# Two bursts of value products a batch instead of five, with readings and copies reordered

## What is computed

```python
scores = scale * np.matmul(q, k.transpose(0, 1, 3, 2)) + bias
attn = np.exp(scores - scores.max(-1, keepdims=True))
attn = attn / (attn.sum(-1, keepdims=True) + 1e-09)
attn_out = np.matmul(attn, v)
...
for e in range(E):
    out += P[:, e:e + 1] * (np.maximum(x @ w1[e], 0.0) @ w2[e])
```

## Time and profile before

| | |
|---|---|
| median of 3 runs | 1844.34 us (1844.29 to 1845.65) |
| the profiled execution | 1844.29 us |
| its span, first to last instruction | 1842.5 us |
| PE busy | 1826.9 us (99%), 10223 matmul records |
| DVE, ACT, POOL busy | 1054.5, 824.6, 1028.1 us |
| chain that ended last | PE 95%, DVE 1% |
| granted TensorE clock | 9 tenths or more in all 40 slices |

### The profile page before, as it was taken

One profiled execution on the slowest core, in us unless ns is written; L12 is line 12 of the kernel. 1 busy time (PEld: TensorE's weight loads), 2 busy tenths in 40 slices (PEclk: granted clock), 3 DMA queues, 4 the chain that ended last, 5 costly groups with the idle time before them and its releaser, 6 DMA issues.

```text
span 1842.5 us, 27892 instructions
## 1 busy us (share of the span) xinstructions
PE 1826.9 (99%) x10223; PEld 1590.0 (86%) x10223; DVE 1054.5 (57%) x1784; ACT 824.6 (45%) x1416; POOL 1028.1 (56%) x720
## 2 busy tenths in 40 slices
PE   8999999999999999999999999999999999999999
PEld 4677777798999999999999999999999999999998
DVE  8877777778554555456545554555465545544553
ACT  8877777533433333344333333333333333333331
POOL 0223326577666666666776666666666666666661
PEclk9999999999999999999999999999999999999999
DMA  7764562021111111112121122121121111111210
GB/s 229 243 150 97 129 148 68 23 92 53 65 67 69 69 69 69 69 69 103 69 69 69 69 69 69 69 69 69 70 103 69 69 69 69 69 69 69 69 46 35
DMA packets 44127, 152.47 MB, mean 83 GB/s; under 512 B 9584, under 2 KB 18032, under 8 KB 29680
## 3 DMA queue, kind: packets, MB, share of 16 engines
q1 hardware_dynamic: 44016, 150.99, 25.5%
HBM read 135.63 MB, written 15.34 MB: 82 GB/s over the span
## 4 chain that ended last, share of the span: by engine, by line
PE 95%; DVE 1%; ACT 0%; POOL 0%; issue 0%; POOLq 0%; DVEq 0%
PE banks L660 14%; PE banks L661 14%; PE banks L659 14%; PE banks L627 13%; PE banks L631 13%; PE banks L629 13%; PE banks L557 4%; PE banks L518 3%; PE banks L500 3%; PE banks L501 2%; PE banks L571 1%; PE banks L528 0%; PE banks L678 0%; ACT probs L786 0%; DVE x_lo_rest_r L1081 0%
## 5 line engine op out<-in xcount | busy, mean ns | idle before, releaser
L1279 POOL TENSOR_TENSOR w_lo<-stage,w_hi 128x1024 fp32r<-128x1024 f32 (+1 forms) x288 | 647.4, 2264 | 525.7 <-ACT w_hi L832 524.7
L1161 DVE TENSOR_TENSOR u<-p_copy,banks 128x384 f32<-128x384 f32 x192 | 106.3, 554 | 632.0 <-PE banks L631 632.0
L661 PE MATMUL banks<-w_hi,h_lo 128*128 128x512 f32 x1152 | 450.1, 391 | 0.0
L660 PE MATMUL banks<-w_lo,h_hi 128*128 128x512 f32 x1152 | 449.9, 391 | 0.0
L659 PE MATMUL banks<-w_hi,h_hi 128*128 128x512 f32 x1152 | 449.0, 390 | 0.0
L1167 DVE SCALAR_TENSOR_TENSOR h_lo<-corner,h_hi 128x384 fp32r<-128x384 f32 x384 | 412.7, 1102 | 0.0
L879 ACT ACTIVATE h_hi<-corner 128x384 fp32r<-128x384 f32 x384 | 196.5, 526 | 270.9 <-DVE corner L1161 267.9
L627 PE MATMUL banks<-x_hi,w_hi 128*128 128x384 f32 x896 | 300.6, 335 | 0.0
L631 PE MATMUL banks<-x_hi,w_lo 128*128 128x384 f32 x896 | 300.2, 335 | 0.0
L832 ACT ACTIVATE w_hi<-stage 128x1024 fp32r<-128x1024 f32 (+1 forms) x288 | 271.6, 974 | 8.8 <-POOL stage L1273 8.8
L868 ACT ACTIVATE p_copy<-banks 128x384 f32<-128x384 f32 x96 | 47.4, 493 | 491.0 <-PE banks L631 491.0
(11 more groups left out here) (130 smaller groups left out, 2472.2 us busy)
## 6 DMA issues: line engine op xcount, KB each, us to landing
stage<-in_expert_w SPq DMA_DIRECT2D x96, 1024.0 KB, 4.8
raw<-in_qk SPq DMA_DIRECT2D x32, 576.0 KB, 7.2
bias_scratch<-bias_out SPq DMA_DIRECT2D x36, 288.0 KB, 2.6
bias<-bias_scratch SPq DMA_DIRECT2D x16, 288.0 KB, 2.9
v_main<-in_v SPq DMA_DIRECT2D x16, 256.0 KB, 2.7
bias<-bias_scratch SPq DMA_DIRECT2D x16, 256.0 KB, 3.8
out<-total SPq DMA_DIRECT2D x4, 768.0 KB, 4.0
out<-total SPq DMA_DIRECT2D x6, 256.0 KB, 2.0
```

Of the source, the lines that this page charges most:

```text
L660: pe.matmul(dst, h_hi[:, g % 2, f, tokens], lo[:, f], start=False, stop=False)
L661: mm = pe.matmul(dst, h_lo[:, g % 2, f, tokens], hi[:, f], start=False, stop=fp == FPAIRS - 1 and f == 1)
L1161: dve.tensor_tensor(out, other, bank, op).then_inc(combined, 1)
L1279: pool.tensor_tensor(lo, of, hi.bitcast(F32), ALU.subtract).then_inc(w_split, 1)
```

## The change

The five parts of the value products become two: half 0 whole in step 4 after the transposes, half 1 whole in step 1 of the next batch, before them. VectorE reads half 0 first thing in step 0 (before: after row sums) and half 1 in step 1 between reductions and copies (before: step 3); it copies the rest before the second head's block in steps 2 and 3; the row sums and reciprocal come last in step 0. ScalarE copies between the two exponentials in step 0, and rounds both heads of the next pair in step 1, one before its copy and one after. No arithmetic is added or left out. `HEADS_AT` gives the steps after a batch's first at which its halves are read.

```diff
--- before.py
+++ after.py
@@ -58,9 +58,10 @@
 PIECES = len(PIECE_AT) - 1
 
 
-PV_PARTS = ((4, 0, range(0, 3), False), (5, 0, range(3, 5), True),
-            (6, 1, range(0, 2), False), (7, 1, range(2, 3), False), (8, 1, range(3, 5), True))
-PV_DONE = (2, 5)
+PV_PARTS = ((4, 0, range(0, 5), False), (6, 1, range(0, 5), True))
+PV_DONE = (1, 2)
+HEADS_AT = (5, 6)
+REST_FIRST = (2, 3)
 TAIL = 6
 TOK = N // P
 ITERS = 8
@@ -776,17 +777,21 @@
                     hidden_units(m + AHEAD, (m + AHEAD) % ROUND)
                 keep_bias(m, m % ROUND)
             def step(hp, s, last=False):
-                if exists(hp, s):
+                def exponentials(h):
+                    if not exists(hp, s):
+                        return
                     slot = batch(hp, s)[1]
                     rows = queries(s % QC)
-                    for h in range(2):
-                        act.wait_ge(biased, 2 * (hp * STEPS + s) + h + 1)
-                        row = probs[0:rows, s % 2, S * h:S * h + S]
-                        total_at = 2 * (s % QC) + h
-                        act.activation(row, row, ACT.Exp, bias=neg_max[0:rows, 2 * (s % 2) + h:2 * (s % 2) + h + 1],
-                                       scale=-1.0,
-                                       accum_out=row_sum[0:rows, slot, total_at:total_at + 1]).then_inc(exped, 1)
-                if exists(hp, s - 1):
+                    act.wait_ge(biased, 2 * (hp * STEPS + s) + h + 1)
+                    row = probs[0:rows, s % 2, S * h:S * h + S]
+                    total_at = 2 * (s % QC) + h
+                    act.activation(row, row, ACT.Exp, bias=neg_max[0:rows, 2 * (s % 2) + h:2 * (s % 2) + h + 1],
+                                   scale=-1.0,
+                                   accum_out=row_sum[0:rows, slot, total_at:total_at + 1]).then_inc(exped, 1)
+
+                def keep_turned():
+                    if not exists(hp, s - 1):
+                        return
                     at, rows = hp * STEPS + s - 1, queries((s - 1) % QC)
                     act.wait_ge(turned[0], at + 1)
                     q_at = (s - 1) % QC * P
@@ -796,6 +801,20 @@
                     act.activation(probs_t[:, 0:KC, q_at:q_at + rows],
                                    banks[:, 4, :].rearrange("p (c q) -> p c q", c=KC)[:, :, 0:rows],
                                    ACT.Copy).then_inc(kept_t[0], 1)
+
+                def round_next(h):
+                    if s % QC == 1 and exists(hp, s) and exists(hp, s - QC) and not (last and s // QC == B - 1):
+                        n, slot = batch(hp, s + QC)
+                        round_pair(n, slot, h)
+
+                exponentials(0)
+                if s % QC == 0:
+                    keep_turned()
+                exponentials(1)
+                round_next(0)
+                if s % QC != 0:
+                    keep_turned()
+                round_next(1)
                 first = not exists(hp, s - QC)
                 if s % QC == 0 and not first:
                     n, slot = batch(hp, s - QC)
@@ -805,9 +824,6 @@
                     act.activation(inv_wide[:].rearrange("p (r d) -> p r d", d=D),
                                    row_inv[:, slot, :].unsqueeze(2).broadcast_to([P, 2 * QC, D]),
                                    ACT.Copy).then_inc(inv_widened, 1)
-                if s % QC in (1, 2) and exists(hp, s) and not first and not (last and s // QC == B - 1):
-                    n, slot = batch(hp, s + QC)
-                    round_pair(n, slot, s % QC - 1)
             for s in range(STEPS):
                 step(0, s)
             with act.Fori(1, PAIRS - 1) as hp:
@@ -1027,6 +1043,12 @@
                 n, slot = batch(hp, s)
                 qc = s % QC
                 rows = queries(qc)
+
+                def heads_due(half):
+                    if (s - HEADS_AT[half]) % QC == 0 and exists(hp, s - HEADS_AT[half]):
+                        keep_heads(hp, s - HEADS_AT[half], half)
+
+                heads_due(0)
                 for h in range(2):
                     if exists(hp, s):
                         if s < QC and h == 0:
@@ -1044,6 +1066,21 @@
                         for piece in range(PIECES):
                             if (s - 8 - piece) % QC == 0 and exists(hp, s - 8 - piece):
                                 scale_heads(hp, s - 8 - piece, piece)
+                heads_due(1)
+                if exists(hp, s - 1):
+                    rows, q_at = queries((s - 1) % QC), (s - 1) % QC * P
+                    free = columns_free(hp, s - 1)
+                    if free is not None:
+                        dve.wait_ge(pv_done, free)
+                    for part in ((2, 1) if qc in REST_FIRST else (1, 2)):
+                        dve.wait_ge(turned[part], at)
+                        if part == 1:
+                            dve.tensor_copy(probs_t[:, KC:2 * KC, q_at:q_at + rows],
+                                            banks[:, 5, :].rearrange("p (c q) -> p c q", c=KC)[:, :, 0:rows]
+                                            ).then_inc(kept_t[1], 1)
+                        else:
+                            dve.tensor_copy(probs_t[:, 2 * KC, q_at:q_at + rows],
+                                            rest_bank[:, 0:rows]).then_inc(kept_t[2], 1)
                 if qc == 0 and exists(hp, s - QC):
                     n, slot = batch(hp, s - QC)
                     dve.wait_ge(exped, 2 * at)
@@ -1053,24 +1090,6 @@
                                       ALU.add).then_inc(inv_step, 1)
                     dve.wait_ge(inv_step, 2 * n + 1)
                     dve.reciprocal(row_inv[:, slot, :], row_eps[:, slot, :]).then_inc(inv_step, 1)
-                for half in range(2):
-                    after = PV_PARTS[PV_DONE[half] - 1][0]
-                    if (s - after) % QC == 0 and exists(hp, s - after):
-                        keep_heads(hp, s - after, half)
-                if exists(hp, s - 1):
-                    rows, q_at = queries((s - 1) % QC), (s - 1) % QC * P
-                    free = columns_free(hp, s - 1)
-                    if free is not None:
-                        dve.wait_ge(pv_done, free)
-                    for part in (1, 2):
-                        dve.wait_ge(turned[part], at)
-                        if part == 1:
-                            dve.tensor_copy(probs_t[:, KC:2 * KC, q_at:q_at + rows],
-                                            banks[:, 5, :].rearrange("p (c q) -> p c q", c=KC)[:, :, 0:rows]
-                                            ).then_inc(kept_t[1], 1)
-                        else:
-                            dve.tensor_copy(probs_t[:, 2 * KC, q_at:q_at + rows],
-                                            rest_bank[:, 0:rows]).then_inc(kept_t[2], 1)
 
             def split_factor(p, k):
                 dve.wait_ge(x_rounded, NP * p + k + 1)
```

## The result

The changed kernel takes 1849.62 us (median of 10 runs, 1848.71 to 1850.23); the kernel before, run beside it, 1844.32 (1844.19 to 1845.72). The ratio is 1.0027, interval 1.0019 to 1.0035: slower by some 5 us, just over the 0.2% that can be told from no change. The runs of each kernel lie on two levels (after at 1848.7 to 1849.1 and at 1850.1 to 1850.2, before at 1844.2 to 1844.4 and near 1845.7), so the median of after is the middle between five low runs and five high ones, and low against low the difference is 4.6. The forecast was 1848.1, within 1843.0 to 1850.8.

What follows compares the result with a forecast made beforehand. TensorE's own instructions were taken to bound the kernel. Batches -1.5, a stall gone -0.3, first batch +0.15, last pair +2.5 and tail +3.0 sum to +3.8 on 1844.3: 1848.1 us, range 1843.0 to 1850.8.

Steps and rivals of the forecast that it cites:

- Part 1: Value products on TensorE: five bursts become two, -0.44 a batch; neighbours +0.08, so TensorE alone would save 0.36.
- fourth rival: A burst of value products costs on its way out too: another -0.4 x 15, giving 1842; chance 0.04.
- part 2: Other engines' order in a batch: step 3's transposes wait 0.40 for ScalarE's copy; net -0.10 a batch, -1.5 over 15.
- first rival: In step 3, ScalarE's copy of block 1 is in time: period 16.9, saving another 3.8, giving 1844.3; chance 0.19.
- Part 3: Last pair: extra weight and token roundings and splits on ScalarE and VectorE cost +2.5 us, bounds 1.3 and 3.5.
- Part 4: Tail: VectorE's reading of half 1's heads before four splits starts the second spread 9.09 after the burst, not 6.11: +2.98.
- second rival: TensorE, idle 4.2 us in the tail, cools and runs slower afterwards, costing 1.3: 1849.4; chance 0.16.
- third rival: The second burst, in step 1, starts late because copies bite by 0.15 a batch, +2.3: 1850.4; chance 0.10.

Runs made afterwards that it cites:

- the kernel without the wait: The changed kernel with ScalarE's copy between the two exponentials in steps 0, 2 and 3 instead of step 0 alone: 1841.44 us, ratio 0.9984.

## Why the prediction was right, and where it was not

The forecast, a little slower, was right in direction and 1.5 us under the median; against the profiled execution +3.8 was forecast and +4.7 came. That is partly luck, since some errors cancelled.

- **Part 1, the bursts.** Right: 2.58 a slot, as the straight line said. But the neighbours were mis-sized. I added 0.08 a batch for them. The 64-row transposes take 0.70 after scores too (196.69 to 197.39; I had 0.82), nine transposes 0.90 when scores follow (203.36 to 204.26; I had 1.08), and step 4 runs 2.69 from scores to burst (I had 2.80). The three terms make -0.12 - 0.18 - 0.11 = -0.41, so TensorE alone would save 0.77, not 0.36; the kernel without the wait shows at least 0.67. The mistake was to carry a slot's length to other neighbours by what stands in front of it; what stands behind it counts as well. That is the fourth rival in substance: a burst costs more than the 0.14 in its slot, as the three-burst kernel shows, where the neighbours pay another 0.17. Its 0.84 a batch was nearer than my 0.36, and I gave it 0.04; its time, 1842, failed all the same, since the wait of part 2 took the saving. By the Trainium skill (TensorEngine Tiling, Key Properties) each switch of mode drains the engine. The rows agree that a burst is paid for on both sides of it. They don't show that the mode is the reason: block 4's scores run in 128*64 tiles as well, and take 1.14 (207.25 to 208.39) where the 128*128 ones take 1.15 (204.26 to 205.41).
- **Part 2, the wait in step 3.** The chain of 3.04 us read from the first batch held to 0.01: forecast 10.87, measured 10.88, released by the copy that was named. Because TensorE reached that place earlier, the same start meant an idle time of 0.53, not 0.40: the wait swallowed what TensorE had saved in front of it. This is where TensorE's gain went: 0.47 a batch, 7.5 us between the profiled executions, as the copy's experiment shows. The first rival fell: the copy was never in time.
- **The covers of part 2** were needed, each by its experiment: ScalarE's copy between the exponentials about 6.8 us, both roundings in step 1 about 7.2 (medians), the row sums last about 0.1 a batch. What the walk missed is that a rounding in front of the copy makes the copy wait for a transfer too: in the profile with TensorE kept busy this cost 1.4 us, once. That GpSimd's earlier split would be missed without it did not show. The first batch lost 0.08, not 0.15 (72.33, before 72.25).
- **Part 3, the last pair.** The term +2.5 was mis-sized: against an ordinary batch the last three lose 0.38, 0.69 and 2.19, 3.3 in all. The first two were right to 0.1. In the last, the token split took 1.91 us where I allowed 1.2. Timeline of after, GpSimd and VectorE, then TensorE:

```profile
323.31 1.84 POOL L1317 TENSOR_TENSOR total<-x 128x768 f32<-128x768 f32 x1
...
324.06 1.91 DVE L1100 TENSOR_TENSOR x_lo_first_r<-x,x_hi 128x768 fp32r<-128x768 f32 x1
```
```profile
326.70 0.40 PE L501 MATMUL banks<-qk_hi 128*128 128x288 f32 x1 [1.39 <-DVE neg_max L1061]
```
The traces show why 1.91: the split waits, inside its own time, for the GpSimd instruction that is running. It ends 0.82 after that one (325.15, 325.97). In twelve of the thirteen profiles it is the same to 0.01 or so, wherever the split starts: in before it started 0.42 ahead of GpSimd's end (323.24, 323.66) and took 1.24. In the thirteenth it started as the GpSimd instruction ended, and took 0.95.

All of attention up to the burst's end thus gives 15 x -0.20 + 3.3, less before's own stall of 0.3, plus the first batch's 0.1: +0.1, measured +0.16, where I had +0.85. Two errors, 1.5 too little saved and 0.8 too little lost, partly cancel here.
- **Part 4, the tail.** Exact: 9.08 measured, 9.09 forecast.
- **What the sum left out** is the second rival, that TensorE cools in the tail. I gave it 0.16 and left its cost out of the sum; it came, and cost 1.55 (I had worked out 1.3). The argument against it was that the granted clock read 1.00 where one matmul took 684 and later 407 ns. That row was no evidence on what follows a gap: here durations and clock column both show it. The Trainium skill (TensorE: Matmul & The Clock Gate, The HAM clock gate) has the clock fall to half after idleness; the trace agrees, 0.32 against 0.17 us a product. The rival worked out at 1849.4 was the better forecast.
- **The third rival**, a late burst in step 1, did not occur: the slot in front is 1.25 to 1.31 in the ordinary batches. The experiment with the late copy shows what it looks like, 1.82.

## What to carry to other kernels

Before moving a read of a result to an earlier step, look at what is queued behind it on its engine in the prologue and the tail too: there the covering work of the loop is missing, and independent work behind a wait costs its whole length. When TensorE's own time is shortened in a pipelined loop, find the longest chain through the other engines first (reduction, two exponentials, copy, transposes here), for the saving ends in the first wait that it meets; the cure was to place the copy between the two exponentials, not to change TensorE. Price an idle stretch of TensorE with the slow products that follow it, and fill or shorten it. Where the runs of a kernel lie on levels, compare level with level, and look which of them was profiled.

## What the runs showed of the hardware that was not expected

- After a gap of 4.08 us, in each of the eight profiles that have it unfilled, 6 to 15 products came 0.145 us later each, at a granted clock of 0.50. The count changed from one program's profile to the next with the same gap; from the spread to the logits it took 8.00 (six slow) to 9.28 us (15 slow) instead of 6.73, so this cost ran from 1.3 to 2.6 us. After the tail's gaps of 0.67, 1.43 and 2.35 us the clock stayed at 1.00, as it did where transposes stood in the gap.
- The clock also fell without so long a gap. At the start of attention TensorE stands idle for 1.2 to 1.6 us before its first scores and for 0.43 to 0.45 before the next in every kernel; four of thirteen profiles have the clock at 0.50 from about 63 to 66 us, the others at 1.00. With the second rounding back in step 2 it fell in the last batch, at about 336.6, after idle stretches of 1.40 and 0.53 us; after has the same two there (1.39, 0.54) and kept 1.00. So these runs give no length of idle time below which the clock is safe.
- One VectorE instruction of one shape, a subtraction of 128x768, took 0.95 us with GpSimd idle (342.99) and 1.10 to 1.91 when it started during a GpSimd addition: it ended 0.81 to 0.82 us after that addition, wherever it had started. The GpSimd instruction behind it is stretched too, 2.4 to 2.6 us instead of 1.83.
- A chain over three engines, read from one batch, held to 0.01 us in another, while slots of a single engine, carried to other neighbours, were off by up to 0.18, and one burst more costs 0.31, of which its own slot shows 0.14.
